# One TensorE visit per chunk in place of two: state and output products beside the next chunk's scores

## What is computed

```python
def _attn_ref(q, k, v, alpha):              # B, H, S, D = 4, 8, 768, 48
    state = np.zeros((B, H, D, D))
    for t in range(S):
        state = alpha[:, :, t, :, None] * state + np.einsum('bhd,bhe->bhde', k[:, :, t], v[:, :, t])
        y[:, :, t] = np.einsum('bhd,bhde->bhe', q[:, :, t], state)

def _moe_ref(x, domain_probs, w1, w2):      # x 3072 x 384, 4 experts, hidden 1024
    p = domain_probs / (domain_probs.sum(-1, keepdims=True) + 1e-09)
    for e in range(E):
        out += p[:, e:e + 1] * (np.maximum(x @ w1[e], 0.0) @ w2[e])

def _moe2_ref(x, w_in, w_out):              # hidden 2048
    h = x @ w_in
    return (h * np.clip(h + 3.0, 0.0, 6.0) / 6.0) @ w_out
```

## Time and profile before

| | us |
|---|---|
| median of three runs | 1395.45 (1394.85 to 1399.09) |
| the profiled execution: time | 1396.57 |
| its span, first to last instruction | 1394.7 |
| PE busy | 1371.8 (98%) |
| DVE, ACT, POOL busy | 698.2, 534.9, 790.4 |
| granted PE clock, mean share of 2.4 GHz | 0.995 |

### The profile page before, as it was taken

The page is one execution under the profiler, slowest core; times in us unless marked ns, Lnnn a source line. Parts: engine busy times, 40 slices in busy tenths (PEclk is TensorE's granted clock), DMA queues, the critical chain, the costliest instruction groups (busy, mean ns, idle before and its releaser), DMA issues.

```text
span 1394.7 us, 31927 instructions
## 1 busy us (share of the span) xinstructions
PE 1371.8 (98%) x12476; PEld 1116.7 (80%) x12476; DVE 698.2 (50%) x1401; ACT 534.9 (38%) x992; POOL 790.4 (57%) x860
## 2 busy tenths in 40 slices
PE   7799999999999999999999999999999999999998
PEld 5578888888888888888888888888888888888887
DVE  8766665445454545454544445454445333333333
ACT  2233333333354333354433335533335433335543
POOL 7866666555655565556555655565555444444442
PEclk9899999999999999999999999999999999999999
DMA  4244333343333433333443333343323343333340
GB/s 144 81 133 117 114 117 107 111 116 103 98 98 121 135 106 113 109 94 114 129 120 105 106 98 117 99 138 104 111 84 94 88 132 100 108 98 95 93 123 34
DMA packets 70659, 150.20 MB, mean 108 GB/s; under 512 B 9584, under 2 KB 22128, under 8 KB 70512
## 3 DMA queue, kind: packets, MB, share of 16 engines
q1 hardware_dynamic: 70512, 148.16, 35.6%
HBM read 143.36 MB, written 4.77 MB: 106 GB/s over the span
## 4 chain that ended last, share of the span: by engine, by line
PE 94%; DVE 0%; issue 0%; ACT 0%; DVEq 0%
PE h_bank L469 42%; PE out_banks L485 29%; PE out_third L485 14%; PE score_banks L395 4%; PE score_banks L433 1%; PE score_banks L441 1%; PE state_bank L416 1%; PE state_bank L406 1%; PE h_bank L449 0%; DVE p_kept L577 0%; DVE result L636 0%; DVE h_bank L616 0%; DVE x_lo L632 0%; ACT gate L748 0%; DVEq L141 0%
## 5 line engine op out<-in xcount | busy, mean ns | idle before, releaser
L858 POOL TENSOR_TENSOR w_lo<-w_raw,w_hi 128x768 fp32r<-128x768 f32 x288 | 531.0, 1844 | 551.5 <-ACT w_hi L761 551.5
L755 ACT ACTIVATE h_hi<-h_bank 128x512 fp32r<-128x512 f32 x288 | 172.5, 599 | 636.2 <-DVE h_bank L610 561.4
L469 PE MATMUL h_bank<-x_hi,w_hi 128*128 128x512 f32 x864 | 336.4, 389 | 0.0
L469 PE MATMUL h_bank<-x_lo,w_hi 128*128 128x512 f32 x864 | 336.1, 389 | 0.0
L469 PE MATMUL h_bank<-x_hi,w_lo 128*128 128x512 f32 x864 | 336.0, 389 | 0.0
L610 DVE SCALAR_TENSOR_TENSOR h_bank<-h_bank,probs 128x512 f32<-128x512 f32 x192 | 134.3, 699 | 356.9 <-PE h_bank L469 356.8
L761 ACT ACTIVATE w_hi<-w_raw 128x768 fp32r<-128x768 f32 x288 | 241.4, 838 | 0.0
L485 PE MATMUL out_banks<-h_hi,w_hi 128*128 128x512 f32 x576 | 232.2, 403 | 0.2 <-DVE x_lo L632 0.2
L485 PE MATMUL out_banks<-h_hi,w_lo 128*128 128x512 f32 x576 | 225.0, 391 | 0.0
L485 PE MATMUL out_banks<-h_lo,w_hi 128*128 128x512 f32 x576 | 224.8, 390 | 0.0
L622 DVE TENSOR_TENSOR h_lo<-h_bank,h_hi 128x512 fp32r<-128x512 f32 x288 | 197.3, 685 | 46.5 <-ACT h_hi L755 46.5
(11 more groups left out here) (76 smaller groups left out, 1210.8 us busy)
## 6 DMA issues: line engine op xcount, KB each, us to landing
w_raw<-w SPq DMA_DIRECT2D x288, 384.0 KB, 3.1
alpha_q<-qa SPq DMA_DIRECT2D x48, 256.0 KB, 3.4
k_raw<-kk SPq DMA_DIRECT2D x48, 128.0 KB, 3.4
probs<-prob_scratch SPq DMA_DIRECT2D x24, 256.0 KB, 3.6
v_diag<-v SPq DMA_DIRECT2D x96, 48.0 KB, 2.4
out<-result SPq DMA_DIRECT2D x18, 256.0 KB, 3.9
level_sb<-level SPq DMA_DIRECT2D x1, 80.0 KB, 3.3
ident_sb<-ident SPq DMA_DIRECT2D x1, 64.0 KB, 3.0
```

Of the source, the lines that this page charges most:

```text
L469: mm = pe.matmul(h_bank[g % 2][:, :], a, x, start=k == 0 and i == 0, stop=k == K3 - 1 and i == 2)
L755: act.activation(h_hi[:, g % DEEP, :], h_bank[g % 2][:, :], ACT.Copy).then_inc(hh_made, 1)
L858: pool.tensor_tensor(w_lo[:, g % RING, :], w_raw[:, g % RAW, :], w_hi[:, g % RING, :].bitcast(F32), ALU.subtract).then_inc(w_lo_made, 1)
```

## The change

The state slot of a chunk becomes the score slot of the next one (only the last chunk, 47, keeps a slot of its own). Both visits of PE are run together in the order: first key transpose of chunk n+1, `carry(n)`, `attend(n)`, `score(n+1)`, second key transpose of n+1. The banks are shared out anew: the attention output goes to `state_bank` columns 192 to 383, the first transpose to its last 128 columns, and the second, which has no bank of its own, goes in two halves of 64 columns to the outer edges of the two score banks, whose slabs of scores shrink from 256 to 224 columns and begin at column 64. It is there written as two ordinary matmuls against halves of the identity. ACT copies the keys in three instructions where it was one, before and not after the weights of that slot. DVE does the state, the output and `x_lo` before it begins to mask the next scores, and the masking waits for the key copies. The chunks of tile 0 keep the old form.

```diff
-SLAB = 256
+SLAB = 224
+SLABS_AT = 64
 def state_slot(n):
-    return score_slot(n) + (2 if n < 2 * PER_TILE else 3)
+    return score_slot(n + 1) if n + 1 < CHUNKS else score_slot(n) + 3
+def turned(n):
+    return carried(n) + max(carried(n) - carried(PER_TILE), 0)
...
-        kt_out = state_bank[:, STATE:STATE + 2 * P]
+        kt_early = state_bank[:, STATE:STATE + 2 * P]
+        kt_first = state_bank[:, 2 * STATE:2 * STATE + P]
+        kt_second = [score_banks[:, 0:SLABS_AT], score_banks[:, 1024 - SLABS_AT:1024]]
...
-            return scores(n)[:, 0:STATE]
+            return scores(n)[:, 0:STATE] if n < PER_TILE else state_bank[:, STATE:2 * STATE]
...  (score)
+                if n > PER_TILE:
+                    pe.wait_ge(keep_made, KEEPS * n)
+                    pe.wait_ge(kn_made, turned(n))
...
+            def turn_k_first(n):
+                pe.wait_ge(k_made, K_STEPS * (n + 1))
+                pe.wait_ge(s_made, carried(n - 1))
+                pe.wait_ge(kn_made, turned(n))
+                pe.wait_ge(x_hi_made, n - 1)
+                pe.wait_ge(x_lo_made, n - 1)
+                pe.transpose(kt_first, k_level(n, LEVELS)[:, 0:2, :], ident_sb[:, :]).then_inc(kt_made, 1)
+            def turn_k_second(n):
+                for i in range(2):
+                    mm = pe.matmul(kt_second[i], k_level(n, LEVELS)[:, 2:4, :], ident_sb[:, own(i)],
+                                   start=True, stop=True)
+                mm.then_inc(kt_made, 1)
...  (attend)
+                if n > PER_TILE:
+                    pe.wait_ge(x_hi_made, n)
+                    pe.wait_ge(x_lo_made, n)
...  (PE, slot g)
                 hidden(g)
-                if g in SCORE_AT:
-                    n = SCORE_AT[g]
-                    score(n)
-                    if not last_of_seq(n):
-                        turn_k(n)
+                n = SCORE_AT.get(g, CHUNKS)
+                turns = n < CHUNKS and not last_of_seq(n)
+                if turns:
+                    turn_k_first(n)
                 if g in STATE_AT:
                     if not last_of_seq(STATE_AT[g]):
                         carry(STATE_AT[g])
                     attend(STATE_AT[g])
+                if n < CHUNKS:
+                    score(n)
+                if turns:
+                    turn_k_second(n)
...  (DVE: keep, next_state and split_x wait for more, slot g)
+                    if n >= PER_TILE:
+                        dve.wait_ge(kn_made, turned(n + 1))
...
-                need(dve, y_made, n)
+                need(dve, y_made, n if n < PER_TILE else n + 1)
...
+                if n >= PER_TILE and n + 1 < CHUNKS and not last_of_seq(n + 1):
+                    dve.wait_ge(kn_made, turned(n + 1) + 1)
...
-                if g in SCORE_AT:
-                    keep_all(SCORE_AT[g], 0, 3)
                 if g in STATE_AT:
                     n = STATE_AT[g]
                     if not last_of_seq(n):
                         next_state(n)
                     turn_y(n)
+                    split_x(n)
+                if g in SCORE_AT:
+                    keep_all(SCORE_AT[g], 0, 3)
                 n, a, b = Q_AT.get(g, (0, 0, 0))
-                for step in range(a, b - 1):
+                for step in range(a, b):
                     scale_q(n, step)
-                if g in STATE_AT:
-                    split_x(STATE_AT[g])
-                if b > a:
-                    scale_q(n, b - 1)
...  (ACT)
+            def copy_k_first(n):
+                act.wait_ge(kt_made, turned(n) + 1)
+                act.wait_ge(kv_made, carried(n))
+                act.wait_ge(y_made, n)
+                act.activation(k_rows[:, 0, :], kt_first, ACT.Copy).then_inc(kn_made, 1)
+            def copy_k_second(n):
+                act.wait_ge(kt_made, turned(n) + 2)
+                for i in range(2):
+                    op = act.activation(k_rows[:, 1, own(i)], kt_second[i], ACT.Copy)
+                op.then_inc(kn_made, 1)
...
-                if g + SPLIT_AHEAD < SLOTS:
-                    weights_hi(g + SPLIT_AHEAD)
                 if g in SCORE_AT:
                     n = SCORE_AT[g]
                     if not last_of_seq(n):
-                        copy_k_rows(n)
+                        copy_k_first(n)
+                        copy_k_second(n)
                     if n + 2 < CHUNKS:
                         odd_k(n + 2)
+                if g + SPLIT_AHEAD < SLOTS:
+                    weights_hi(g + SPLIT_AHEAD)
```

More of the change, by code:

```diff
@@ L372, in score @@
                 j_out = scores(n)
-                need(pe, x_hi_made, n - 1 if n < PER_TILE else n)
-                need(pe, x_lo_made, n - 1 if n < PER_TILE else n)
+                need(pe, x_hi_made, min(n, PER_TILE) - 1)
+                need(pe, x_lo_made, min(n, PER_TILE) - 1)
+                if n > PER_TILE:
+                    pe.wait_ge(keep_made, KEEPS * n)
+                    pe.wait_ge(kn_made, turned(n))
                 pe.wait_ge(in_qa[n % QRING], 16 * (n // QRING + 1))
@@ L393, in score @@
                                         "p (m r x) -> p m r x", r=2, x=1 << l)[:, :, 1, :]
-                                lo = 512 * i + SLAB * jp + at
+                                lo = SLABS_AT + SLAB * (2 * i + jp) + at
                                 mm = pe.matmul(j_out[own(jj), lo:lo + width], k_level(n, l)[own(i), j, :], moving,
@@ L405, in turn_k @@
                 for jp in range(2):
-                    mm = pe.transpose(kt_out[:, jp * P:(jp + 1) * P], k_level(n, LEVELS)[:, 2 * jp:2 * jp + 2, :],
+                    mm = pe.transpose(kt_early[:, jp * P:(jp + 1) * P], k_level(n, LEVELS)[:, 2 * jp:2 * jp + 2, :],
                                       ident_sb[:, :])
+                mm.then_inc(kt_made, 1)
[10 more added lines that the diff above has]
+                                   start=True, stop=True)
                 mm.then_inc(kt_made, 1)
@@ L412, in carry @@
                 pe.wait_ge(in_v[n % 2], 32 * (n // 2 + 1))
-                pe.wait_ge(kn_made, carried(n) + 1)
+                pe.wait_ge(kn_made, turned(n + 1))
                 for jp in range(2):
@@ L556, in keep @@
             def keep(n, step):
-                s = scores(n)[:, :].rearrange("p (a c) -> p a c", c=SLAB)
+                s = scores(n)[:, SLABS_AT:SLABS_AT + 4 * SLAB].rearrange("p (a c) -> p a c", c=SLAB)
                 dst = p_kept[:, :, :, :].rearrange("p i a t -> p (i a) t")
@@ L725, in copy_k_rows @@
                 need(act, kv_made, carried(n))
-                act.activation(k_rows[:, :, :].rearrange("p a n -> p (a n)"), kt_out, ACT.Copy).then_inc(kn_made, 1)
+                act.activation(k_rows[:, :, :].rearrange("p a n -> p (a n)"), kt_early, ACT.Copy).then_inc(kn_made, 1)
+            def copy_k_first(n):
[8 more added lines that the diff above has]
+                op.then_inc(kn_made, 1)
             def decay_state(n):
@@ L838, in scale_k @@
                 if l == LEVELS - 1:
-                    need(pool, kt_made, carried(n - 1))
+                    need(pool, kt_made, turned(n - 1))
                 pool.wait_ge(k_made, K_STEPS * n + l)
```

## The result

The changed kernel takes 1408.6 us, the median of six runs (1407.6 to 1411.2). The kernel before took 1397.1 beside it (1394.9 to 1399.1). The ratio is 1.0088, with a 95% interval of 1.0078 to 1.0099. The forecast was 1403.0, slower by 7.5 us, with 1409 as the upper end of the range; it is slower by 11.5. The sign was right, and a third of the loss was not foreseen.

The account below looks back on a forecast made before the run. PE's own queue was taken as the bound. 35 merged visits at +0.22 us (+7.7), four at -0.16 (-0.6) and slot 0 (+0.4) gave +7.5 on the median 1395.45: 1403.0 us, range 1398.5 to 1409.

Parts of the forecast that it names:

- The wait ahead of the scores: Merged visit, before the scores: two more semaphores make PE's sequencer late, +0.06 us, with 0 and 0.17 as ends.
- a slack that only later slots have: DVE's `h_lo` after a merged visit: of 4.3 us of slack before PE needs it, about 3.5 stay, so no cost.
- The waits of PE should still be near nothing: Sign to check in PE's waits: any row of several us would make the forecast wrong.
- the sequencer's case: Rival, ahead of the scores: sequencer falls behind for good, wait 0.17 not 0.06 us, +4.3, 1407.3 us; chance 0.11.
- 4 visits with nothing to turn: Merged visits whose new chunk is the last of a sequence: -0.22 + 0.06 = -0.16 us each, -0.6 together.
- slot 0's visit: Score visit with nothing to merge: +0.11 + 0.44 - 0.17 = +0.4 us.
- The edges: Between large and small matmuls: a merged pair loses one way out and one way in, -0.22 us.
- the head: Start of the visit: the first key transpose moved there costs +0.11 us, bounds 0 and 0.20.
- the tail: End of the visit: two old transposes go, -0.17 us; the second returns as ordinary matmuls, four weight loads, +0.44.
- short loads: Rival, visit's tail: ordinary loads as quick as the transposes' (0.055 us), tail 0.22, waits ahead, 1392.6 us; chance 0.08.
- that rule: Rival, visit's tail: the four loads and streams run serially, 0.66 us, +7.9 more, 1410.9 us; chance 0.05.
- own range 1399 to 1406: Range of the forecast case itself, from the wait's 0 to 0.17 and the head's 0 to 0.20 us; chance 0.66.

Follow-up runs that it names:

- e2: The changed kernel with the second key transpose as two half transposes (64 partitions each) in place of ordinary matmuls: 1398.3 us.
- e1: The changed kernel with the nine semaphore waits of the scores moved ahead of the first key transpose: 1404.3 us.
- e7: e5 with DVE making `h_lo(0)` ahead of chunk 8's masking and `h_lo(1)` ahead of the query steps: 1391.9 us, 0.9968 of the kernel before.
- e4: The changed kernel with its banks, copies and tail, but state visits two or three slots behind their score visit as before: 1412.0 us.
- e8: The kernel before with only the second key transpose, from chunk 8 on, written as two fp32 products with the identity: 1408.4 us.
- e6: e3 with 42 small products of zeros added at PE's start: 1398.6 us.
- e3: The changed kernel with the edits of e1 and e2 together: 1398.1 us.
- e5: e3 with four small products of zeros added at PE's start: 1393.7 us.

## Why the forecast was right in its sign and short in its size

Three steps failed. The wait ahead of the scores was put at 0.06 us a visit and measured 0.12. The supply of instructions to PE was put at nothing, without being looked at, and took 3.0 us in one profile and 1.6 in the other. DVE's lateness in the first two slots was put at nothing, by a slack that only later slots have, and took 1.2 us. The prediction had named the sign of this, "The waits of PE should still be near nothing", and PE's waits are where it showed. That 1408.6 lies inside 1398.5 to 1409 is in part luck: the upper end was there for the sequencer's case, which did not come as described, and the three steps above filled the room.

The slots grew by 13.8 us in the first profile of the changed kernel and by 12.3 in the second. Term by term:

```
                                              forecast   1st    2nd
35 visits: edges, tail, head                    +5.6     +5.6   +5.6
4 visits with nothing to turn                   -0.9     -0.9   -0.9
slot 0's visit                                  +0.4     +0.4   +0.4
waits ahead of the scores                       +2.3     +4.3   +4.1
PE out of instructions                            0      +3.0   +1.6
first two slots, late h_lo                        0      +1.2   +1.2
sum                                             +7.5    +13.6  +12.0
```

**The edges, the head, the tail.** Right to a hundredth of a microsecond each. L443 stood 279.89 - 279.46 = 0.43 behind the last large matmul, as written down. In this visit the tail took 0.468 from its start to the large matmul, of which 0.023 come back, since the next one follows in 0.313 where it took 0.336: 0.445, against 0.44. This term rested on the earlier trace rows, a load of the same kind far away in the prelude. The other side of the range, short loads at 0.22, was the price of a transposed tail, which e2 has (0.18 by the same reckoning).

The Trainium skill, "TensorE: Matmul & The Clock Gate", Part 3 ("The mechanism"), says that a weight load overlaps matmuls in flight only where its row group differs; by that rule the tail was put at 0.66. The trace does not agree: four loads and four streams of the full array took 0.445, and the loads started 0.11 apart, so loads passed under streams of the same rows.

**The waits: the mechanism was right, the size not.** The term read "four wait instructions from 0.13 on", 0.13 + 0.44 = 0.57, and then took off "a few hundredths" because the last wait would overlap its successor. It does not. They began at 0.13, took 0.107 each, and the scores followed 0.11 behind the last: 0.56 at best, 0.577 on average. Nothing held the correction but a guess. Beyond the join, some 0.02 a visit is spread over the large matmuls behind it, gone in e1 with the join; why is open.

The ranges were sloppy as well. The forecast's "own range 1399 to 1406" was to follow from the wait's 0 to 0.17 and the head's 0 to 0.20. Both low ends together give 1403.0 - 39 x 0.06 - 36 x 0.11 = 1396.7, both high ones 1403.0 + 39 x 0.11 + 36 x 0.09 = 1410.5, and the wait's 0.17 was the sequencer rival's price too, so it was counted under two chances.

**The sequencer rival.** It had the sequencer fall behind for good. It was on the right road: a long row of small records was named as the danger ("157 small records come in a row where at most 98 did"), but as a matter of queueing in front of the engine. What ran dry lay one step further back, the supply of instructions to the sequencer. The prediction has no term for it. The page's line of the instruction queue, 0.5% of sixteen engines, looks like nothing; the share is small because the packets are few, and what counts is the 2.2 to 3.2 us from one's start to its use.

**The other engines: the slack was taken from a full slot.** "PE needs it for `hidden(g + 2)`, behind three groups of nine large matmuls" holds from slot 2 on. In slots 0 and 1 there is no `project` yet, so between the visit and `hidden(2)` lies one group, not three, and there the 1.93 us that DVE waited for ACT's copies had no cover. Everywhere else it had: DVE waited 36.1 us in all for these copies, and PE did not notice. Counted from the visit's end, the masking and `h_lo` ran when the prediction had them: at the visit above, which ends at 283.39, DVE's masking starts at 284.09 and `h_lo` ends at 285.92, T + 2.5 where T + 2.6 stood. e7 shows that both waits go when `h_lo` comes first.

**What it means for the change.** Merging itself gains: 0.10 a pair, by e4 against the changed kernel, and more with the waits ahead. The products that came with it took 12 us (e8), the waits 4, the first transpose at the head 0.11 a visit. With transposes of half height, waits ahead, the count shifted and DVE's order mended, it is 0.3% ahead of the kernel before (e7).

## What to carry to other kernels

Price a move of PE's work by start-to-start times of the same instruction form elsewhere in the trace: here such terms were right to 0.01 us, while the one term with a guessed correction was off by half. When small instructions are gathered into one run, count them: past 300 in a row, at 9 ns each, PE could outrun the delivery of its own program, and whether it does depends on where the packet borders fall, so a time of such a kernel can move by 4 us with sixteen instructions at its start. And where a wait is hidden by work of neighbouring slots, look at the first and last slots, in which that work is missing.

## What the runs showed of the hardware that I had not expected

**PE's instruction packets.** Where PE stood for one, it went on 2.2 to 3.2 us after the packet had begun (22 of the 27 stalls in seven profiles lie between 2.2 and 2.7) and 1.3 to 1.6 us after its recorded transfer had ended. Each of the 27 stood at record 256k + 449 with packet k the last begun, less than two packets' 512. Products of 64x64 tiles ran 300 records in 2.7 us. The Trainium skill, "Runtime: NRT & Kernel Launch", section "Instruction fetch mechanics", says the program is refilled in blocks of 256 instructions, with PE's store holding 2048 of them, and that the fetch is hidden because dispatch is slower than the fill. The block's size is what the runs show. A store of 2048 does not fit stalls at record 449; the store of two blocks that the section gives for the other engines would. And the fetch was not hidden: in runs at 9 ns a record PE stood for up to 1.5 us.

**The clock once fell behind such a stall.** In e6 PE stood for 1.2 us at 1010.3 us, and then ran at a granted clock of 0.57 from 1011.9 to 1015.9, with matmuls 0.425 us apart where 0.227 is usual, the 1.2 GHz level:

```profile
1011.90:1015.90 4.00, 4.00 (x13) 3.12 (x12) 1.76 (x4) 1.27 (x4) 1.83 (x1) 0.57 0.02 5
```

In e3 it stood equally long at 729 us, and the clock stayed at 1.00 behind it:

```profile
730.50:734.50 4.00, 4.00 (x21) 3.26 (x20) 1.76 (x4) 1.28 (x4) 1.84 (x1) 1.00 0.45 129
```

Behind the stall, the next 79 records took 9.33 us in e6 and 7.76 in e5: that one fall cost about 1.6 us on top of its stall. What decides between the two cases, no run here shows.
